# Top-k attention and two gated MLPs on one core: the two score tiles of a unit together, an older unit's value products right behind them, MLPs one slot later

## What is computed

```python
scores = scale * np.matmul(q, k.transpose(0, 1, 3, 2))
kth = np.partition(scores, -top_k, axis=-1)[..., -top_k:-top_k + 1]   # top_k = 32
scores = np.where(scores >= kth, scores, -1000000000.0)
attn = np.exp(scores - np.max(scores, axis=-1, keepdims=True))
attn = attn / (np.sum(attn, axis=-1, keepdims=True) + 1e-09)
x = np.matmul(attn, v)                      # then to [2304, 512]
gate = 1.0 / (1.0 + np.exp(-(x @ w_gate)))  # 512 -> 1536
y = gate * (x @ w_val) @ w_out              # 1536 -> 512
h = np.maximum(y @ w_in, 0.0)               # 512 -> 2048
out = (h * h) @ w_out2                      # 2048 -> 512
```

## Time and profile before

| | us |
|---|---|
| median of 3 runs | 1272.64 (1272.38 to 1274.31) |
| the profiled execution, device time | 1273.17 |
| its span in the trace | 1271.4 |
| PE busy in it | 1205.5 (95%) |
| DVE busy | 849.6 (67%) |
| ACT busy | 738.5 (58%) |
| POOL busy | 626.0 (49%) |

### The profile page before, as it was taken

One profiled execution on the slowest core, in us unless ns is written; L12 is line 12 of the kernel. 1 busy time (PEld: TensorE's weight loads), 2 busy tenths in 40 slices (PEclk: granted clock), 3 DMA queues, 4 the chain that ended last, 5 costly groups with the idle time before them and its releaser, 6 DMA issues.

```text
span 1271.4 us, 21720 instructions
## 1 busy us (share of the span) xinstructions
PE 1205.5 (95%) x7520; PEld 986.7 (78%) x7520; DVE 849.6 (67%) x1756; ACT 738.5 (58%) x1758; POOL 626.0 (49%) x539
## 2 busy tenths in 40 slices
PE   3679999699999999999999999999999999999999
PEld 1458877588888878888887777777777777888999
DVE  7989988478779967878986667688854544710121
ACT  5877767467668656656765665567544344531221
POOL 4875668456558634544653444356523342540220
PEclk9999999899999999999999999999999999999999
DMA  7785666677565675554555655445555545556997
GB/s 266 271 309 192 235 205 223 212 278 252 194 239 205 234 254 188 195 183 151 181 189 188 206 176 180 168 160 168 183 167 186 176 166 174 168 177 209 354 365 270
DMA packets 89245, 270.13 MB, mean 212 GB/s; under 512 B 9904, under 2 KB 15024, under 8 KB 89136
## 3 DMA queue, kind: packets, MB, share of 16 engines
q1 hardware_dynamic: 89136, 268.74, 61.9%
HBM read 228.33 MB, written 40.37 MB: 211 GB/s over the span
## 4 chain that ended last, share of the span: by engine, by line
PE 78%; POOL 9%; ACT 6%; issue 3%; DMA 3%; SPq 1%; DVE 1%; ACTq 0%; POOLq 0%; DVEq 0%
PE ps L481 22%; PE ps L483 19%; PE ps L482 19%; PE ps L422 6%; PE ps L389 5%; PE ps L402 4%; POOL below L706 4%; POOL ring L701 3%; PE ps L467 2%; DMA w_split<-ring 2%; POOL probs L711 1%; ACT probs L530 1%; ACT ring L557 1%; ACT below L516 1%; ACT scores L511 1%
## 5 line engine op out<-in xcount | busy, mean ns | idle before, releaser
L706 POOL TENSOR_TENSOR below<-scores,below 128x576 f32<-128x576 f32 x144 | 204.7, 1422 | 366.4 <-ACT below L523 365.9
L639 DVE MAX8 top<-work 128x8 f32<-128x576 f32 x432 | 313.0, 752 | 5.0
L481 PE MATMUL ps<-xy_hi,ring 128*128 128x512 f32 (+3 forms) x800 | 298.2, 373 | 16.8 <-POOL xy_lo L717 16.8
L483 PE MATMUL ps<-xy_hi,ring 128*128 128x512 f32 (+3 forms) x800 | 284.3, 355 | 0.0
L482 PE MATMUL ps<-xy_lo,ring 128*128 128x512 f32 (+3 forms) x800 | 283.7, 355 | 0.0
L641 DVE MATCH_REPLACE8 work<-top,work 128x576 f32<-128x576 f32 x288 | 213.8, 743 | 0.0
L481 PE MATMUL ps<-g_hi,ring 128*128 128x512 f32 (+3 forms) x560 | 207.2, 370 | 0.0
L481 PEld LDWEIGHTS ps<-xy_hi,ring 128*128 128x128 f32 x800 | 151.8, 190 | 60.2 <-issue 27.3
L483 PE MATMUL ps<-g_hi,ring 128*128 128x512 f32 (+3 forms) x560 | 198.1, 354 | 0.0
L482 PE MATMUL ps<-g_lo,ring 128*128 128x512 f32 (+3 forms) x560 | 197.6, 353 | 0.0
L665 DVE SCALAR_TENSOR_TENSOR full_buf<-act_buf,ps 128x512 f32<-128x512 f32 (+3 forms) x60 | 35.6, 594 | 199.4 <-PE ps L483 199.3
(11 more groups left out here) (56 smaller groups left out, 1717.4 us busy)
## 6 DMA issues: line engine op xcount, KB each, us to landing
ring<-w_split SPq DMA_DIRECT2D x318, 512.0 KB, 3.9
w_split<-ring SPq DMA_DIRECT2D x68, 512.0 KB, 4.2
ring<-w_in SPq DMA_DIRECT2D x113, 256.0 KB, 3.5
vt<-v_in SPq DMA_DIRECT2D x16, 480.0 KB, 5.2
heads_in<-qk_in SPq DMA_DIRECT2D x16, 336.0 KB, 4.6
vt<-v_in SPq DMA_DIRECT2D x16, 320.0 KB, 4.0
heads_in<-qk_in SPq DMA_DIRECT2D x16, 240.0 KB, 3.9
heads_in<-qk_in SPq DMA_DIRECT2D x8, 368.0 KB, 4.7
```

The costliest lines, as they stand in the source:

```text
L481: nc.tensor.matmul(dst, w_hi, hi[:, k, 0:WIDTH[c]], start=first, stop=False)
L483: mm = nc.tensor.matmul(dst, w_lo, hi[:, k, 0:WIDTH[c]], start=False, stop=final)
L639: nc.vector.max(out=best, in_=sc if step == 0 else wk).then_inc(sel_step[t % 2], 1)
L706: nc.gpsimd.tensor_tensor(out=below[:, t % 2, :], in0=scores[:, t % 4, :], in1=below[:, t % 2, :], op=ALU.subtract).then_inc(mask_done, 1)
```

## The change

Scores no longer come one tile a slot. `SCORE_AT` names the slot in which a unit is scored, three slots before its first tile is needed, and both of its tiles are scored there one after the other. Tiles that are the second of a unit (part 1) go to banks 2 and 3, the banks of the turns; the others stay in banks 0 and 1. For that a part-1 score waits for the copies of all turns in earlier slots, and a turn waits for the copies of all part-1 scores up to its own slot. ACT copies both tiles at the start of the slot after their score. The buffer `scores` has six places in place of four.

In a slot the order on PE is now: part 0, the scores, the products, parts 1 and 2 of the MLP halves, the turn. ACT empties part 0's blocks, then copies the products, then empties part 1's. The MLPs of chunks 1 to 5 begin one slot later (16, 41, 69, 101, 133, 149), and there are 150 slots. The loads of `heads_in` are issued a slot earlier. `pe_ns` counts 1300 ns for a pair of scores and 700 for a half unit's.

```diff
-MLP_AT = [CHUNK_END[c] + 5 for c in range(NC)]
+MLP_AT = [CHUNK_END[c] + (6 if c else 5) for c in range(NC)]
+PLACES = 6
+SCORE = 3
+FIRST_OF = [min(t for t in range(NT) if TILES[t][0] == u) for u in range(NU)]
+SCORE_AT = {FIRST_OF[u] - SCORE: u for u in range(NU)}
...
-        scores = sb("scores", [P, 4, SEQ])
+        scores = sb("scores", [P, PLACES, SEQ])
...
-        def s_ps():
-            return ps[:, 0:2, 0:HALF]
+        def score_bank(t):
+            return 2 if TILES[t][1] == 1 else 0
...
-                wait(pe, s_copied, t)
+                wait(pe, s_copied, FIRST_OF[u])
+                if part == 1:
+                    wait(pe, pt_copied, sum(END[v] + TURN < FIRST_OF[u] - SCORE for v in range(NU)))
...
             def turn(u):
                 pe.wait_ge(norm_done, END[u] + 1)
                 wait(pe, pt_copied, u)
+                wait(pe, s_copied, max([t + 1 for t in range(NT) if TILES[t][1] == 1
+                                        and FIRST_OF[TILES[t][0]] - SCORE <= END[u] + TURN], default=0))
...
             for s in range(SLOTS):
                 for c, h in SHARES[s][0]:
                     mlp_half(c, h)
-                if s + 2 < NT:
-                    score(s + 2)
-                for c, h in SHARES[s][1]:
-                    mlp_half(c, h)
+                if s in SCORE_AT:
+                    for t in tiles_of(SCORE_AT[s]):
+                        score(t)
                 if s - PROD in UNIT_AT:
                     times_v(UNIT_AT[s - PROD])
-                for c, h in SHARES[s][2]:
+                for c, h in SHARES[s][1] + SHARES[s][2]:
                     mlp_half(c, h)
                 if s - TURN in UNIT_AT:
                     turn(UNIT_AT[s - TURN])
...
-                wait(act, mask_done, t - 3)
+                wait(act, mask_done, t - PLACES + 1)
...
-            for s in range(SLOTS):
-                if s + 1 < NT:
-                    copy_scores(s + 1)
+            for s in range(min(SCORE_AT) + 1, SLOTS):
+                if s - 1 in SCORE_AT:
+                    for t in tiles_of(SCORE_AT[s - 1]):
+                        copy_scores(t)
...
-                for c, n in blocks_of(SHARES[s][0] + SHARES[s][1]):
+                for c, n in blocks_of(SHARES[s][0]):
                     evac(c, n)
                 if s - PROD in UNIT_AT:
                     copy_x(UNIT_AT[s - PROD])
+                for c, n in blocks_of(SHARES[s][1]):
+                    evac(c, n)
```

More of the change, by code:

```diff
@@ L110 @@
 MASK, NORM, TURN, PROD = 2, 3, 3, 4
-MLP_AT = [CHUNK_END[c] + 5 for c in range(NC)]
+MLP_AT = [CHUNK_END[c] + (6 if c else 5) for c in range(NC)]
[3 more added lines that the diff above has]
+SCORE_AT = {FIRST_OF[u] - SCORE: u for u in range(NU)}
 SLOTS = MLP_AT[NC - 1] + 1
 def pe_ns(s):
-    t, u, v = s + 2, UNIT_AT.get(s - TURN), UNIT_AT.get(s - PROD)
+    t, u, v = SCORE_AT.get(s), UNIT_AT.get(s - TURN), UNIT_AT.get(s - PROD)
+    scored = 0 if t is None else 700 if UNITS[t][4] else 1300
     turned = 0 if u is None else 550 if UNITS[u][4] else 980
     products = 0 if v is None else 800 if UNITS[v][4] else 1300
-    return (800 if t < NT else 0) + turned + products
+    return scored + turned + products
 def shares():
@@ L140, in shares, with tiles_of @@
     return out
+def tiles_of(u):
+    return [t for t in range(NT) if TILES[t][0] == u]
 SHARES = shares()
@@ L160 @@
 for _g in range(2, NG):
-    HEADS_AT.setdefault(max(FIRST_TILE[_g - 1] - 2, 0), []).append(_g)
+    HEADS_AT.setdefault(max(FIRST_TILE[_g - 1] - 3, 0), []).append(_g)
 for _c in range(1, NC):
@@ L388, in score @@
                         r = 2 * (g % 2) + h
-                        mm = nc.tensor.matmul(ps[out_rows, half, 0:HALF], heads_in[rows, r, P * i:P * i + n],
+                        mm = nc.tensor.matmul(ps[out_rows, score_bank(t) + half, 0:HALF], heads_in[rows, r, P * i:P * i + n],
                                               heads_in[rows, r, q:q + HALF], start=True, stop=True)
@@ L487, in _ @@
             pe.wait_ge(const_ready, 1)
-            score(0)
-            score(1)
+            for s in range(min(SCORE_AT), 0):
+                if s in SCORE_AT:
+                    for t in tiles_of(SCORE_AT[s]):
+                        score(t)
             for s in range(SLOTS):
@@ L508, in copy_scores @@
             def copy_scores(t):
-                wait(act, mask_done, t - 3)
+                wait(act, mask_done, t - PLACES + 1)
                 act.wait_ge(s_scored, t + 1)
-                nc.scalar.activation(two(scores[:, t % 4, :]), s_ps(), ACT.Copy).then_inc(s_copied, 1)
+                bank = score_bank(t)
+                nc.scalar.activation(two(scores[:, t % PLACES, :]), ps[:, bank:bank + 2, 0:HALF], ACT.Copy).then_inc(s_copied, 1)
             def find_below(t):
                 act.wait_ge(sel_step[t % 2], 7 * (t // 2 + 1))
-                nc.scalar.activation(below[:, t % 2, :], scores[:, t % 4, :], ACT.Sign,
+                nc.scalar.activation(below[:, t % 2, :], scores[:, t % PLACES, :], ACT.Sign,
                                      bias=top[:, t % 4, TOPK - 1:TOPK], scale=-1.0).then_inc(sign_done, 1)
@@ L602, in _ @@
             nc.scalar.activation(rsum_eps[:, 0:1], ident[:, 0:1], ACT.Exp)
-            copy_scores(0)
-            for s in range(SLOTS):
-                if s + 1 < NT:
-                    copy_scores(s + 1)
+            for s in range(min(SCORE_AT) + 1, SLOTS):
+                if s - 1 in SCORE_AT:
+                    for t in tiles_of(SCORE_AT[s - 1]):
+                        copy_scores(t)
+                if s < 0:
+                    continue
                 if 0 <= s - MASK < NT:
@@ L629, in select @@
             def select(t, step):
-                sc, wk, tp = scores[:, t % 4, :], work[:, t % 2, :], top[:, t % 4, :]
+                sc, wk, tp = scores[:, t % PLACES, :], work[:, t % 2, :], top[:, t % 4, :]
                 if step == 0:
@@ L705, in mask @@
                 pool.wait_ge(below_done, t + 1)
-                nc.gpsimd.tensor_tensor(out=below[:, t % 2, :], in0=scores[:, t % 4, :], in1=below[:, t % 2, :],
+                nc.gpsimd.tensor_tensor(out=below[:, t % 2, :], in0=scores[:, t % PLACES, :], in1=below[:, t % 2, :],
                                         op=ALU.subtract).then_inc(mask_done, 1)
```

## The result

| | before | after |
|---|---|---|
| median of the runs, us | 1273.47 (4 runs, 1272.38 to 1274.70) | 1251.98 (4 runs, 1251.24 to 1252.19) |
| ratio, 95% interval | | 0.983 (0.9813 to 0.9847) |
| span of the profiled execution | 1271.4 | 1250.4 |
| PE busy | 1205.5 | 1169.2 |

The change is faster by 21.5 us. The forecast was 1246, the range 1230 to 1262.

A forecast was written before the change was run, and what follows sets the result against it. PE, busy for 95% of the span, was taken to bound the kernel, above all from 274.3 to 1169.6 us. 1273.2 - 27.7 - 7.3 - 3.5 + 12.0 = 1246.7, forecast as 1246, range 1230 to 1262.

The forecast's parts named there:

- PE's work: From 274.3 to 1169.6 us, fewer changes of matmul shape and moved work were to save 27.7 us, from 21 to 34.
- the direct step: On PE, products right behind a score save one of two shape changes: 0.19 us each, 6.3 us in 33 runs.
- The later MLPs: First blocks of chunks 2 to 5: four PE waits for `xy_lo` (5.7 us) and a clock fall (1.6) go, 7.3 together.
- Added waits: Turns and part-1 scores waiting on PE for ACT's copies were to cost 12 us, bounds 2 and 25.
- the four slots from 56 to 63: Chunk 1 slots where ACT lags behind PE; their turn waits counted as largest lag 4.3 plus 2 us.
- The rival in which ACT keeps ahead: ACT reaches the banks sooner, turns' waits come to 2 us: 1236, or 1228 if the store chain gives way; chance 0.17.
- The 29 slots: Slots from 41 on where a turn waits for its own slot's part-1 score copies; nine were to show a wait.
- the slower rival: ACT late in every shared slot, each of 29 turns waiting 2.0 us: 58 us in place of 12, 1292; chance 0.07.
- wait (a): A part-1 score waits for copies of the turn one slot earlier; claimed covered by MLP work, except 0.2 us in chunk 0.
- Before the first MLP block: Before 89.6 us DVE paces everything and the change gives it nothing to do or skip: no gain, no loss.
- Chunk 0 and the step to chunk 1: Stores still end chunk 0 near 240, slot 40's turn is done at 249: gain 3.5 us, bounds 0 and 12.
- The signs of being wrong: Pairs over 1.6 us, turns waiting in chunks 2 and 3 as well, or MLP blocks beginning to wait for ACT or DVE.

## Why the prediction was right, and where it was not

- **PE's work (-27.7).** Right, and by its own steps. A pair costs 1.38 us against 1.37, pair and products 2.61 against 2.62, and taking the direct step back cost 6.2 us, waits and clock taken out, against 6.3. No run takes the pairs apart again; their 17 us are read from the timeline and from the sum of the stretch. 4.2 of the 27.7 us only moved ahead of the stretch.
- **The later MLPs (-7.3).** The four waits and the fall of the clock went, as said. That the edit alone shortened the long stretch by 7.3 us is luck: new waits took 2.3 us of it, and 3.3 us of work had moved out. Of the 5.7 us, 0.7 lie in the last chunk's MLPs.
- **Added waits (+12.0).** Mis-sized. Behind 284.7 they came to 5.0 us. The step that failed was counting the four slots from 56 to 63 at ACT's largest lag, 6.3 us: only the turn of slot 61 waited there, 1.95 us. The rival in which ACT keeps ahead is nearer for this stretch. That it skips a copy in the slots between is my explanation; no run isolates it. Two smaller things were wrong. The 29 slots are 22 in the kernel's order: in the other seven a half unit is scored, whose tile goes to banks 0 and 1, for which no turn waits. That is 1.0 of the 12 us, and 14 of the 58 in the slower rival. And wait (a) was not always covered: in chunk 2's MLPs it once took 1.5 us.
- **Before the first MLP block (0).** Wrong. "DVE paces everything" nearly held in the kernel before, where DVE waited 1.7 us for ACT's `rsum_eps` in these slots; the step that failed was to conclude that the change leaves this alone. It made those waits 5.9 us. Two of the added waits bite there as well (slots 11 and 13, 7.6 us), where no MLP work stands between a score and a turn of the same slot, and the prediction had looked for them only from slot 41 on. It cost 5.9 us, 2.6 of them by the waits.
- **Chunk 0 and the step to chunk 1 (-3.5).** The mechanism was right: the chain of stores paces chunk 0, and the turn of slot 40 waits for copies behind a split that waits for a load. The size was not: the gain came out as a loss of 4.5 us, 8 worse. The turn was to be done at 249; it was at 257.7, of which 5.9 us are the late start handed on and 2.8 a chain no faster than before (chunk 0's own work was through at 248, 153 us after its first block, where I had 150). From there to chunk 1's 8th block I had 22 us and it took 27.0. The sum put no wait of PE in it, but the turn of slot 42 waited 3.9 us for the same reason as that of slot 40 (2.0 of them stood in the 12 us above).
- **Slower (0.07)** needed over 38.5 us of added waits. In the whole span PE waited 22.2 us for score copies before a turn, in 7 places.
- **The signs of being wrong.** Two came in a small way without deciding the time: one turn waited 1.1 us in chunk 3's MLPs (slot 125), and MLP blocks waited 3.8 us in all for ACT or DVE, where it had been 2.8.

The Trainium skill (TensorEngine Tiling (Array Packing), Key Properties) had it that a change of tiling mode drains TensorE. The trace agrees as far as it can show: scores followed directly by products still pay one change, 0.2 us.

## What to carry to other kernels

Where an engine is busy throughout, count how often its kind of work changes and what a change costs, and group like with like: here a change of matmul shape cost 0.2 us, and 119 changes fewer in the long stretch (two for each of 43 pairs, one for each of 33 direct steps) were some 23 of its 30.4 us. Grouping makes longer waits elsewhere: each resource that is now shared needs its release early in the releasing engine's order, ahead of anything that can wait for a DMA. And a stretch paced by a chain in an in-order queue takes little part in a gain until the queue's wait is moved: asking for a load one block later gave 12 to 14 us here, with the change or without it. Count all waits of such a queue, as the next one in order takes over most of what the first gives up: 45 us less for stores were 12.7 in all. And count the work in a stretch before and after, lest work that moved over its border be taken for a gain.

## What the runs showed of the hardware that was not expected

The profile's clock row can miss a stretch at the lower level. In the kernel before it says 1.00 up to 85 us:

```profile
75.00:85.00 10.00, 6.50 (x33) 4.55 (x35) 9.43 (x21) 7.76 (x20) 8.37 (x7) 1.00 0.77 236
```

Yet in these 10 us a score tile takes 1.33 us (at 81.78), where one takes 0.76 at 602.22, and every full tile ahead of it takes 1.33 as well. The change shows the same up to 34 us: the row says 1.00, and a turn at 28.97 takes 2.18 us, where one takes 1.15. For the whole of the first stretch the rows say 0.99 before and 0.79 after, though it is in the kernel after that some single tiles ran in 0.76 us there (at 36.57, 38.47, 54.15 and 56.06). Comparing the durations of one kind of matmul told more than the row.
